# Attention and two expert layers on one core: small inputs prepared two steps earlier, difference blocks of a plain step regrouped

## What is computed

```python
def reference(q, k, v, moe, moe2):
    # attention; 576 positions, head dim 64, stride 32
    scores = q @ k.T / 8
    scores = where(mask_local if head < 4 else mask_strided, scores, -1e9)
    x = softmax(scores) @ v                      # -> 1152 tokens x 512
    # layer 1: one expert of 8 for each token, 512 -> 1024 -> 512
    logits = x @ w_gate + modality_bias[modality_id]
    e = argmax(logits); g = softmax(logits)[e]
    x = g * (relu(x @ w1[e]) @ w2[e])
    # layer 2: all 4 experts for every token, 512 -> 1024 -> 512
    p = domain_probs / (domain_probs.sum(-1) + 1e-9)
    return sum(p[:, e] * (relu(x @ u1[e]) @ u2[e]) for e in range(4))
```

## Time and profile before

| | before |
|---|---|
| median of 3 runs | 647.75 us (647.41 to 647.89) |
| the profiled execution, its own time | 647.75 us |
| its span, first to last instruction | 645.7 us |
| TensorE, matmuls busy | 611.2 us (95%) |
| VectorE busy | 354.1 us (55%) |
| GpSimd busy | 301.3 us (47%) |
| ScalarE busy | 207.0 us (32%) |

### The profile page before, as it was taken

How to read it: one execution, slowest core, us unless ns; L and a number is a source line. 1 busy time by engine, 2 the same in 40 slices (tenths; PEclk the granted TensorE clock), 3 DMA queues, 4 the chain that set the end, 5 groups by cost and what they waited for, 6 DMA issues and landing times.

```text
span 645.7 us, 10625 instructions
## 1 busy us (share of the span) xinstructions
PE 611.2 (95%) x3665; PEld 535.3 (83%) x3666; DVE 354.1 (55%) x687; ACT 207.0 (32%) x529; POOL 301.3 (47%) x280
## 2 busy tenths in 40 slices
PE   5999667999999999999999999999999999999995
PEld 4888655678876788989988988998998998998894
DVE  5887726852248522368455455545545555545653
ACT  3865306642246422213212312311321321231230
POOL 6543371016000000662999685576576568557005
PEclk9999697999999999999999999999999999999999
DMA  9917153784105201100211110120110111010003
GB/s 231 232 23 261 62 192 133 279 300 157 51 16 213 81 16 32 40 27 1 66 66 65 66 36 32 65 65 2 65 65 16 49 65 32 32 65 0 0 0 147
DMA packets 25650, 54.05 MB, mean 84 GB/s; under 512 B 6680, under 2 KB 9368, under 8 KB 25624
## 3 DMA queue, kind: packets, MB, share of 16 engines
q1 hardware_dynamic: 16904, 28.78, 14.3%
q0 software_dynamic: 6848, 21.52, 9.6%
q10 hardware_dynamic: 1872, 3.41, 1.7%
HBM read 48.70 MB, written 5.00 MB: 83 GB/s over the span
## 4 chain that ended last, share of the span: by engine, by line
PE 79%; issue 5%; DVE 5%; POOL 3%; SPq 3%; ACT 1%; ACTq 1%; DMA 1%; another core or an unknown queue 0%; DVEq 0%; POOLq 0%
PE bank L1267 29%; PE bank L1238 28%; PE bank L1194 8%; PE bank L1206 7%; PE bank L1178 1%; POOL out L516 1%; DVE w_lo L895 1%; SPq L322 1%; PE bank L1072 1%; DMA dprob<-in_moe_domain_probs 1%; DVE w_lo L901 1%; PE bank L1125 1%; ACT w_hi L564 1%; PE bank L1093 1%; PE bank L1172 1%
## 5 line engine op out<-in xcount | busy, mean ns | idle before, releaser
L978 DVE SCALAR_TENSOR_TENSOR acc<-bank,meta_s,acc 128x512 f32<-128x512 f32 x135 | 100.8, 748 | 62.2 <-PE bank L1267 62.1
L1267 PE MATMUL bank<-u_hi,h_hi 128*128 128x512 f32 x288 | 112.2, 390 | 0.0
L1267 PE MATMUL bank<-u_lo,h_hi 128*128 128x512 f32 x288 | 112.1, 389 | 0.0
L1267 PE MATMUL bank<-u_hi,h_lo 128*128 128x512 f32 x288 | 112.0, 389 | 0.0
L465 POOL CAST u_hi<-u_raw 128x1792 fp32r<-128x1792 f32 (+1 forms) x16 | 25.6, 1598 | 107.3 <-PE bank L1238 102.8
L1025 DVE SCALAR_TENSOR_TENSOR h_lo<-bank,h_hi 128x288 fp32r<-128x288 f32 x112 | 50.9, 454 | 44.7 <-ACT h_hi L662 23.0
L1238 PE MATMUL bank<-x2T_hi,u_hi 128*128 128x288 f32 x232 | 68.4, 295 | 0.0
L1238 PE MATMUL bank<-x2T_lo,u_hi 128*128 128x288 f32 x232 | 68.4, 295 | 0.0
L1238 PE MATMUL bank<-x2T_hi,u_lo 128*128 128x288 f32 x232 | 68.3, 295 | 0.0
L1238 PE MATMUL bank<-t_hi,u_hi 128*128 128x288 f32 x224 | 66.2, 295 | 0.0
L1238 PE MATMUL bank<-t_lo,u_hi 128*128 128x288 f32 x224 | 66.0, 295 | 0.0
(11 more groups left out here) (194 smaller groups left out, 1256.3 us busy)
## 6 DMA issues: line engine op xcount, KB each, us to landing
w_raw<-in_moe_w SPq DMA_DIRECT2D x10, 2048.0 KB, 8.2
u_raw<-in_moe_w POOLq DMA_DIRECT2D x16, 512.0 KB, 3.7
u_raw<-in_moe_w POOLq DMA_DIRECT2D x16, 256.0 KB, 3.1
u_raw<-in_moe_w POOLq DMA_DIRECT2D x32, 128.0 KB, 2.8
x_tile<-x_by_rank ACTq DMA_DIRECT2D x13, 256.0 KB
qT<-in_qT SPq DMA_DIRECT2D x4, 576.0 KB, 8.3
kT<-in_kT SPq DMA_DIRECT2D x8, 288.0 KB, 10.1
v_rows<-in_v_by_position SPq DMA_DIRECT2D x12, 128.0 KB, 10.9
```

What stands on the lines that cost most here:

```text
L978: w.scalar_tensor_tensor(out=acc[:, t, :], in0=bank[Z_BANK[i]][:], scalar=meta_s[:, t, bass.ds(e + 1, 1)], in1=acc[:, t, :], op0=ALU.mult, ...
L1267: last = t_.matmul(bank[Z_BANK[i]][:], lhs[:, c, ts], rhs[page][:, c, :], start=c == 0 and k == 0, stop=c == 1 and k == 2)
```

## The change

There are three edits, on VectorE and ScalarE; TensorE, GpSimd and SP have the same instructions in the same order.

```diff
@@ VectorE, attention @@
             for i in range(STEPS + LAG_V):
-                if i == TILES + 2:
+                if i == TILES:
                     small_steps()
@@ VectorE, plain steps @@
-            dve.wait_ge(meta_in, 16)
-            w.tensor_copy(out_row[:], meta_s[:, :, 0]).then_inc(out_rows_known, 1)
             cut_plain(0, 0)
...
             for j in range(1, len(PLAIN_ORDER)):
                 cut_plain(0, j)
+            dve.wait_ge(meta_in, 16)
+            w.tensor_copy(out_row[:], meta_s[:, :, 0]).then_inc(out_rows_known, 1)
...
             for j in range(len(PLAIN_ORDER)):
-                if j in (0, 3):
-                    dve.wait_ge(x_summed, 2 * DC * (1 if j == 0 else 2))
+                if j % 4 == 0:
+                    dve.wait_ge(x_summed, 2 * DC * (j // 4 + 1))
                     for at in order_t:
-                        make_t(0 if j == 0 else 1, *at)
+                        make_t(j // 4, *at)
                 cut_plain(1, j)
-                if j in (1, 4):
+                if j % 4 == 2:
                     for at in order_t:
-                        split_t(0 if j == 1 else 1, *at)
+                        split_t(j // 4, *at)
@@ ScalarE, plain step 1 @@
                 keep_plain(1, j)
-                if j == 3:
+                if j == 5:
                     act.wait_ge(t_split[0], 4)
-                if j in (0, 3):
+                if j % 4 == 1:
                     for at in sorted(T_AT, key=T_AT.get):
-                        cut_t(0 if j == 0 else 1, *at)
+                        cut_t(j // 4, *at)
```

## The result

The changed kernel takes 666.28 us (median of 4, 665.55 to 669.34) where the kernel before takes 647.82 beside it: a ratio of 1.0286, interval 1.0244 to 1.0327, or 18.5 us more. I had forecast 655.8 and a range to 658.6. The direction was right, the size was less than half of the truth, and the time lies outside the range.

The account below looks back on a forecast made before the run. TensorE, busy for 95% of the span, was taken as the bound. The sum was 647.75 + 4.3 (stall) + 2.0 (clock) + 1.75 (plain step 1) = 655.8 us, range 652.8 to 658.6.

Parts of the forecast that it names:

- Edit 2: Plain step 0: moving the cast of out_row from ahead of the first cut to behind the eighth costs nothing.
- Edit 1, the stall: Attention: small VectorE block two steps earlier waits for dprob's load, delaying TensorE's step-10 flip; 4.3 us, bounds 3.9 to 4.8.
- Edit 1, the clock: Attention behind TensorE's 4.7 us gap: clock falls, 3 to 6 us of work runs slow; costs 2.0 us.
- allowance of 1.3 us for the later low stretches: Two later low-clock stretches may change length when shifted: 1.3 us either way in the range, nothing in the sum.
- Edit 3: Plain step 1: regrouped t blocks end the last split_t later, delaying GpSimd's sums and TensorE; 1.75 us, bounds 1.2 to 2.4.
- (b): Rival: low clock behind attention's gap lasts 10 us and more, losing 4.6 us and more; 658.4 and up, chance 0.10.
- (d): Rival: attention's small loads land by 30.66, so the earlier block costs nothing and a 0.49 us stall goes; 649.0, chance 0.04.

Follow-up runs that it names:

- fill1: Kernel before with the small block two steps earlier, plus 20 unused matmuls in TensorE's gap ahead of step 10's flip: 648.60 us against 644.62, ratio 1.0054.
- early1: Kernel before with the small block two steps earlier and the four small loads issued from ScalarE's queue at the start: 646.92 us, ratio 1.0039.
- cast_mid: Kernel before with the cast of out_row behind the fourth cut of plain step 0: 645.52 us, run once.

## Why the prediction was wrong, point by point

- **Edit 2 is the step that failed.** "The cast of out_row ... Nothing either way" was argued from waits alone: who waits for whom, and what lands when. All of that was right, and it left out that a cast from SBUF to SBUF on VectorE stands still beside GpSimd. It cost 9.4 us alone (8.5 in the trace of that run, 9.0 in the changed kernel's), and the miss is 10.5. None of the rivals had it either. "The new place is ahead of the first sum of z, which waits for TensorE" looked at the slack of VectorE and not at what was running on the neighbour: GpSimd's sums start at 273.19 in the kernel before, and the eighth cut is done at 275.08.
- **The trace of before had shown it**, in rows that I passed over. Three small instructions of attention are longer than their kind. Timelines of VectorE and GpSimd before:

```profile
38.99 0.27 DVE L764 TENSOR_SCALAR neg_max<-row_max 126x4 f32<-126x4 f32 x1
...
41.90 0.71 DVE L737 TENSOR_TENSOR r<-logits,lmax 128x8 f32<-128x8 f32 x1
42.64 0.17 DVE L738 TENSOR_TENSOR r<-r,e_down 128x8 f32<-128x8 f32 x1
...
47.27 0.84 DVE L747 TENSOR_TENSOR order_tmp<-run_no,order_tmp 128x8 f32<-128x8 f32 x1
```

```profile
38.20 1.03 POOL L425 TENSOR_TENSOR prob<-prob,row_inv 126x504 f32<-126x504 f32 x1 [3.19 <-DVE row_inv L773]
...
41.56 1.03 POOL L425 TENSOR_TENSOR prob<-prob,row_inv 126x504 f32<-126x504 f32 x1 [0.67 <-DVE row_inv L773]
...
47.06 1.04 POOL L425 TENSOR_TENSOR prob<-prob,row_inv 96x512 f32<-96x512 f32 x1 [2.03 <-DVE row_inv L773]
```

L764 ends at 39.26 and GpSimd at 39.23, L737 at 42.61 and GpSimd at 42.59, L747 at 48.11 and GpSimd at 48.10. Eight columns take 0.71 or 0.84 us, and the same form 0.17 a moment later (L738). The Trainium skill, page SBUF — State Buffer, section "Who interferes with whom", says that VectorE and GpSimd share a pair of SBUF ports, and that where an instruction of each needs it, the one that issues first holds it for its whole instruction while the other blocks. These rows agree; the 10.38 us go beyond it, since the cast is held not for one sum but to the end of the run of them.
- **Edit 1, the stall: right.** The place and the release chain came out as forecast, the times of the chain within 0.3 us and the wait within 0.5. The forecast was 4.3 us; fill1 gives 4.3 by its trace and 3.5 (2.0 to 5.0) by its times.
- **Edit 1, the clock: right in kind, a little small.** 2.0 us forecast, with bounds of 1.4 to 2.7; 2.3 to 2.7 by the traces, about 3 by the times. The second low stretch, 2.7 us in the trace after, was not foreseen at its place: the allowance of 1.3 us for the later low stretches took their lengths from a routing that waits for other engines, and this one falls on attention work.
- **Edit 3: the mechanism right, the term too large.** 1.75 us forecast; 1.35 on GpSimd's release, 1.2 more on TensorE's gap (1.33 less 0.14), and 1.4 from plain step 0 to the end in both traces. The range of 1.2 to 2.4 held. The row that differs is ScalarE's first casts: 2.38 us in the trace after, where I took 2.62, since all four differences were ready when they began.
- **Together** edits 1 and 3 were forecast at 8.05 us and measured at 7.3 (5.2 to 9.3).
- **The rivals.** The low clock that lasts (b) did not come behind edit 1's gap: behind the flip at 39.04 it was at 0.50 to about 44.6. A second low stretch came 27 us later, and kernels without edit 1 can have that one too. Loads that land in time (d) were built in early1, and the cost went, as (d) said it would.
- **The range** was made from the terms that I had priced. A term at zero had no range at all, and that is where the miss lay.

## What to carry to other kernels

When an instruction moves, ask what the neighbour engine does at the new place, not only who waits for whom; here the price between VectorE and GpSimd was the rest of the unbroken run that the instruction met, and it was charged to whoever waited for VectorE. A short instruction whose duration is several times that of its kind in a trace marks such a hold: compare its end with the end of GpSimd's. A zero in a sum needs bounds like any other term. And a gap on TensorE can cost more than its length where TensorE bounds the stage: here about 2.5 us on top of a stall of 4.3 and, as far as the trace shows, 2.1 on top of 6.9. A sum that ends in a stretch which repeats to 0.1 us is better checked there than on the whole time.

## What the runs showed of the hardware that I had not expected

- A VectorE instruction with all its inputs in SBUF, of 9 or of 288 columns, took 10.35 to 10.64 us when it met sixteen GpSimd sums issued back to back, 9.15 when it met them a little later, 4.37 when the run was cut to eight, 2.00 against one instruction. With 9 columns it ended within 0.05 us of GpSimd's last instruction each time, with 288 columns 0.33 us behind it. GpSimd did not slow down meanwhile: its sixteen sums took 12.13 us with VectorE held and 12.28 without. It did in the one case where VectorE came in between two sums (1.33 us instead of 0.80).
- Instructions with an input from a PSUM bank kept their 0.46 and 0.75 us beside the same run, and ScalarE's cast took 0.20.
- The granted clock fell inside gaps of 4.2 us (attention) and 6.9 us (the z products) and was at 1.2 GHz for about 5 us of work behind both. Filling the first gap with unneeded matmuls kept it at 2.4 GHz (fill1). In the last turns of attention the clock fell in some executions and not in others, of kernels with the same attention (before and cast_mid).
